# Three products in place of four to turn the rows of an mLSTM chunk

## The reference

```python
for t in range(S):
    m_new = np.maximum(f_gate[:, :, t] + m, i_gate[:, :, t])
    f_stab, i_stab = np.exp(f_gate[:, :, t] + m - m_new), np.exp(i_gate[:, :, t] - m_new)
    C = f_stab * C + i_stab * outer(v_t, k_t);  n = f_stab * n + i_stab * k_t
    y[:, :, t] = sigmoid(o_gate_t) * (C @ q_t) / np.maximum(np.abs(n . q_t), 1.0)
x = y as (B * S, H * D)                    # 1536 tokens x 320
g = x @ w_in;  x = (g - np.tanh(g)) @ w_out
out = sum over e of p[:, e] * (np.maximum(x @ w1[e], 0) @ w2[e])
```

## Time and profile before

| | |
|---|---|
| three runs | 600.75, 601.23, 603.22 us, median 601.23 |
| the profiled execution | 598.93 us, of which span 597.2 us |
| PE busy | 590.5 us (99%), 3688 products |
| PEld / DVE / ACT / POOL busy | 538.3 / 237.0 / 196.0 / 103.1 us |
| granted TensorE clock | 0.9 or more of full in all of the 40 slices, mean 1.0 |
| DMA | 37.52 MB, mean 63 GB/s |

### The profile page before, as it was taken

One profiled execution on the slowest core, in us unless ns is written; L12 is line 12 of the kernel. 1 busy time (PEld: TensorE's weight loads), 2 busy tenths in 40 slices (PEclk: granted clock), 3 DMA queues, 4 the chain that ended last, 5 costly groups with the idle time before them and its releaser, 6 DMA issues.

```text
span 597.2 us, 8879 instructions
## 1 busy us (share of the span) xinstructions
PE 590.5 (99%) x3688; PEld 538.3 (90%) x3688; DVE 237.0 (40%) x474; ACT 196.0 (33%) x389; POOL 103.1 (17%) x74
## 2 busy tenths in 40 slices
PE   8999999999999999999999999999999999999998
PEld 7899999988888899999999999999999999999997
DVE  6667756665654643423131313131313131313222
ACT  5775544435432455531113311113311111111111
POOL 3968111001000035620002410004400000000000
PEclk9999999999999999999999999999999999999999
DMA  6976443302000013320001210001000000001011
GB/s 257 363 250 237 153 153 105 99 5 105 1 2 1 0 49 115 127 98 1 1 1 49 98 49 0 1 1 48 1 1 0 2 1 0 1 1 44 1 44 46
DMA packets 10630, 37.52 MB, mean 63 GB/s; under 512 B 1294, under 2 KB 3166, under 8 KB 10590
## 3 DMA queue, kind: packets, MB, share of 16 engines
q1 hardware_dynamic: 10590, 36.95, 17.8%
HBM read 34.92 MB, written 2.02 MB: 62 GB/s over the span
## 4 chain that ended last, share of the span: by engine, by line
PE 95%; DVE 3%; issue 1%; ACT 1%; DMA 0%; SPq 0%; DVEq 0%
PE bank L955 11%; PE bank L956 11%; PE bank L957 11%; PE bank L1005 9%; PE bank L1006 9%; PE bank L1007 9%; PE bank L958 5%; PE bank L959 5%; PE bank L976 4%; PE bank L978 4%; PE bank L977 3%; PE bank L833 3%; PE bank L822 2%; PE bank L984 2%; PE bank L985 2%; PE bank L840 2%
## 5 line engine op out<-in xcount | busy, mean ns | idle before, releaser
L799 DVE SCALAR_TENSOR_TENSOR g_lo<-bank,g_hi 128x512 fp32r<-128x512 f32 x96 | 66.4, 692 | 253.5 <-ACT g_hi L560 253.5
L560 ACT ACTIVATE g_hi<-bank 128x512 fp32r<-128x512 f32 x96 | 57.5, 599 | 269.8 <-PE bank L959 269.8
L1005 PE MATMUL bank<-w_all,g_hi 128*128 128x320 f32 x384 | 118.6, 309 | 0.0
L1007 PE MATMUL bank<-w_all,g_lo 128*128 128x320 f32 x384 | 118.3, 308 | 0.0
L1006 PE MATMUL bank<-w_all,g_hi 128*128 128x320 f32 x384 | 118.2, 308 | 0.0
L955 PE MATMUL bank<-x_hi,w_all 128*128 128x512 f32 (+2 forms) x318 | 118.1, 371 | 0.1
L956 PE MATMUL bank<-x_lo,w_all 128*128 128x512 f32 (+2 forms) x318 | 118.0, 371 | 0.0
L957 PE MATMUL bank<-x_hi,w_all 128*128 128x512 f32 (+2 forms) x318 | 117.7, 370 | 0.0
L393 POOL TENSOR_TENSOR w_all<-w_raw,w_all 128x1408 fp32r<-128x1408 f32 x16 | 51.8, 3234 | 228.5 <-ACT w_all L454 228.5
L1005 PEld LDWEIGHTS bank<-w_all,g_hi 128*128 128x128 f32 x384 | 72.0, 188 | 3.7
L1006 PEld LDWEIGHTS bank<-w_all,g_hi 128*128 128x128 f32 x384 | 72.1, 188 | 3.5
(11 more groups left out here) (118 smaller groups left out, 654.6 us busy)
## 6 DMA issues: line engine op xcount, KB each, us to landing
w_raw<-in_w SPq DMA_DIRECT2D x24, 704.0 KB, 4.1
feat<-in_feat SPq DMA_DIRECT2D x12, 512.0 KB, 5.7
tok<-in_tok SPq DMA_DIRECT2D x12, 484.0 KB, 6.2
zb<-z SPq DMA_DIRECT2D x10, 512.0 KB, 4.5
out<-arena SPq DMA_DIRECT2D x12, 160.0 KB, 1.9
g_tmp<-in_gates SPq DMA_DIRECT2D x1, 64.0 KB
z<-zr SPq DMA_DIRECT2D x1, 56.0 KB, 7.0
g_tmp<-in_gates SPq DMA_DIRECT2D x1, 48.0 KB
```

Of the source, the lines that this page charges most:

```text
L560: A(g_hi[:, b, 0:N], h_ps[b][:, 0:N], ACT.Relu).then_inc(ghi_ready, 1)
L799: V.scalar_tensor_tensor(g_lo[:, b, 0:N], h_ps[b][:, 0:N], 0.0, g_hi[:, b, 0:N].bitcast(F32), ALU.max, ALU.subtract).then_inc(g_ready, 1)
L1005: mm(out, g_hi[:, b, t], high_w, start=first, stop=False)
L1007: last = mm(out, g_lo[:, b, t], high_w, start=False, stop=stop)
```

## The change

`yt` has 64 more columns in each slot. For chunks 2 to 11 VectorE, after the write of the rows, waits for it and copies the tail (columns 256 to 319) behind them (columns 320 to 383); only this copy tells TensorE and SP that the rows are there (`y_ready`). TensorE then turns columns 256 to 383 in one product of 128 columns, which gives the tail twice, and leaves the fourth product out. Chunks 0 and 1 stay as they were.

```diff
-        yt = sb("yt", [P, 2, D])
+        yt = sb("yt", [P, 2, D + TAIL])
...
-                V.scalar_tensor_tensor(yt[:, n % 2, :].rearrange("p (h d) -> p h d", d=HD), o, 1.0, y,
-                                       ALU.add, ALU.mult).then_inc(y_ready, 1)
+                rows = yt[:, n % 2, 0:D]
+                last = V.scalar_tensor_tensor(rows.rearrange("p (h d) -> p h d", d=HD), o, 1.0, y, ALU.add, ALU.mult)
+                if n >= BATCH:
+
+                    chain.done(last)
+                    chain.wait()
+                    last = V.tensor_copy(yt[:, n % 2, D:D + TAIL], rows[:, 2 * P:D])
+                last.then_inc(y_ready, 1)
...
-                nc.tensor.transpose(t_ps[:, 2 * P:3 * P], src[:, D - P:D], ident[:, :])
-                nc.tensor.transpose(t_ps[0:TAIL, 2 * P:3 * P], src[:, 2 * P:D], ident[:, :]).then_inc(t_ready, 1)
+                if n < BATCH:
+                    nc.tensor.transpose(t_ps[:, 2 * P:3 * P], src[:, D - P:D], ident[:, :])
+                    last = nc.tensor.transpose(t_ps[0:TAIL, 2 * P:3 * P], src[:, 2 * P:D], ident[:, :])
+                else:
+                    last = nc.tensor.transpose(t_ps[:, 2 * P:3 * P], src[:, 2 * P:D + TAIL], ident[:, :])
+                last.then_inc(t_ready, 1)
```

## The result

Twenty runs each: 602.77 us after (600.85 to 605.47) against 600.79 before (598.81 to 603.24). The ratio is 1.0032, 95% interval [1.0017, 1.0046], that is 1.9 us. The changed kernel once more, with eleven runs, gave 1.0025 [1.0010, 1.0040].

The account below looks back on a forecast made before the run. TensorE was taken to bound the kernel, with 95% of the chain of waits. Terms 1.15 + 1.35 + 0.1 - 0.66 gave +1.9 us on the three-run median of 601.23, so 603.2 us, range 599.7 to 604.7.

Parts of the forecast that it names:

- The product saved: TensorE's turn, chunks 2 to 11: one product less, 0.11 us each, kept in six chunks, 0.66 us.
- The copy's own cost: VectorE's new copy of 128 x 64 behind the write of the rows: 0.19 us, bounds 0.17 and 0.22.
- L627's speed: A contiguous VectorE operation, 286 ns for 128 elements, read as a mode using both of VectorE's ways into SBUF.
- case 1: Copies of chunks 2 and 3 held by POOL's running operation: +1.9 us, 603.2 us; chance 0.60.
- case 2: Copy not held by POOL in any chunk: -0.57 us, 600.7 us; chance 0.33.
- L622, the witness against: A VectorE COPY of 96 elements in short pieces, 253 ns, full price per element; taken as evidence against a hold.
- Room on VectorE: About 0.14 us of added VectorE time fits in chunks 5 to 11; in chunks 2 to 4 later steps slip 0.1 us.
- The hold: Copies starting beside POOL's L382 wait for its end: loss 1.15 us in chunk 2, 1.35 us in chunk 3.
- the pattern of L689: A VectorE operation beside POOL's took 1.17 us, not 0.49; so a held copy ends 0.05 behind POOL.
- TensorE's wait in front of the scores of chunk 4: Sign for the profile after: TensorE waits over 1 us for L697, VectorE's state, before these scores.
- The rule weighed: 2-port copies and GpSimd operations block each other fully: with this rule +1.9 us, without it -0.57.
- Rival 3: Held copies' pauses let TensorE's clock fall from 2.4 to 1.2 GHz: 1.9 us more, 605.1 us; chance 0.07.

Follow-up runs that it names:

- e3: The changed kernel with chunks 2 and 3 done the old way too, so copies and three products only from chunk 4 on; ratio to before 1.0001.
- e4: The changed kernel with the tail copied by a TENSOR_REDUCE over an axis of length 1 in place of the COPY; ratio to before 1.0003.
- e0_again: The changed kernel once more, unchanged; ratio to before 1.0025.
- e8_again: Second run of the changed kernel with the copy's 64 columns written in permuted order, destination in steps of 8; ratio to before 1.0031.

## Why the prediction was right

**The product saved** was put at 0.11 us, kept in six of ten chunks, 0.66 us. D2 and the rest, which hold the turns of chunks 5 to 11, gave 0.50, so this term was 0.16 too large. The price of 0.11 is right where products are narrow: from one write of rows to the next, 16.18 became 16.07 in chunks 5, 6 and 7. In chunks 9, 10 and 11 it was 0.08, 0.02 and 0.06. There products of 512 columns run, and some of their distances have grown a little (the eight of L965 behind chunk 10's rows by 0.03 together); why, stays open. In chunks 3, 4 and 8 the saving was lost in the waits, as said: the turn of chunk 8 is inside a distance of 29.95 us in both kernels. In chunk 2 the prediction counted the saving as part of the loss; by the run with only the copies, which loses the same there with four products, there was none to be had.

**The copy's own cost** was put at 0.19 us with 0.17 and 0.22 as bounds; it is 0.195. The argument for it stood on L627's speed and was right in its result. The next step, from that speed to the way that is shared with GpSimd, is not shown: the permuted copy has the full price and is held all the same, so a copy's speed did not decide between case 1 and case 2. That case 1 came true is owed in part to luck. L622, the witness against, was none: by this run its slowness says nothing of a hold.

**Room on VectorE.** None lost in chunks 5 to 11, as worked out. In chunk 4 the distance to the next rows grew by 0.09 (predicted 0.1). The delay of VectorE is there as worked out, but the same delay left 0.01 in the run with only the copies, so that the agreement to 0.01 is partly chance.

**The hold.** By the pattern of L689 the copies were to end 0.05 behind POOL's end; they end 0.05 and 0.04 behind. Chunk 2 was put at +1.15 and measured at +1.08 (13.64 against 12.56 from rows to rows), chunk 3 at +1.35 and measured at +1.34 (12.38 against 11.04). The experiments tie both to the meeting with L382: without the meeting (e3) or without the COPY (e4) D1 falls by 2.4 us, and with half of L382 the hold is less than half. Two smaller things were off. The loss of chunk 2 was written as 1.15 us where its own times give 1.17 (38.62 - 37.45). And of the signs named for the profile after, TensorE's wait in front of the scores of chunk 4 did not come as told: it is 0.35 us for L703 (the old L697) and not over 1 us, because the turn of chunk 3 needs the held copy as well, and TensorE waits 0.89 us for it there. The prediction had this turn done before; the distance between the rows came out the same, since VectorE sets it.

**The sum** was +1.9 us, the traces give +2.0, the runs +1.9. The time itself was forecast as 603.2 us and measured as 602.8: the median of three runs from which it started, 601.23, was 0.4 above that of twenty.

**The rule weighed.** The Trainium skill (SBUF — State Buffer, Who interferes with whom) has copies and tensor-with-scalar operations in a 2-port mode block with GpSimd's for the whole instruction, and `tensor_reduce` never. For the copy and the reduce the runs agree, at 1.43 and 0.22 us; no run has such an operation with a scalar start beside GpSimd's, or a GpSimd operation held by a copy. The Trainium skill (VectorE: DVE Perf Modes, What auto-detection actually checks) would have the permuted copy in the faster mode, since its outermost counts are even. The run agrees in the hold (1.46 us) and not in the price (0.226 against 0.195).

**Rival 3**, the falling clock, had 0.07 with a price of 1.9 us. It does happen, in two of five profiled executions, at 1.4 us. What failed there is the form of the rival, all or nothing for the kernel; it is a matter of the single execution. If two in five held for the timed runs too, their mean loss would be 2.6 us, ratio 1.0043; the three ratios of kernels with both holds and three products (1.0032, 1.0025, 1.0031) speak for fewer. So does the granted clock of the timed runs: its mean is 0.9951 over the 21 runs of e0_again and e8_again and 0.9946 over the 21 of before beside them, where two in five would have put the former 0.0011 below the latter. On the other side a clock of 0.991 or 0.992 stands beside 6 of 48 runs of kernels with both pauses and beside 5 of 148 without, so that how often it happens stays open.

## What to carry to other kernels

Before a VectorE copy from SBUF to SBUF goes between a result and the engine that waits for it, look at what GpSimd does at that moment: here the copy's price became what was left of GpSimd's running operation and 0.05 us. The same bytes can go by an operation that isn't held (here a reduce over an axis of length 1, at 0.025 us more) or be computed twice out of PSUM. And a product less is worth its distance in the chain only where no wait stands behind it: here ten products of 0.11 us gave 0.55. And a change of 0.1% is better read from distances in the trace, or from runs of equal granted clock, than from the medians of all runs.

## What the runs showed of the hardware that the prediction did not have

- The hold ends between two POOL operations that follow without a gap: with halves of about 1.0 us the copy got in after the first (0.62 us in all).
- A copy at the full price per element (0.226 us for 64 columns) is held like a fast one (0.195).
- The stage of low clock between 5 and 25 us puts the rows of chunk 2 at 38.3 us and later in place of 36.15 where it lasts 6.8 us, and at 36.8 to 37.4 where it lasts 3.4 us. The timed runs of one kernel scatter with their mean granted clock (before: 599.0 us at 1.00, 601.0 at 0.994).
- The same pauses, up to 1.2 us from product to product, were followed by a fall of the clock in two executions and by none in three. What tells them apart, and whether the pauses are the cause, stays open.
